# One attention, mixing and MLP kernel: the order of a batch's end, who adds the transform to x, where a row norm's inverse root stands, which engine step splits which weight when, and a 64-column transpose of the last key tile

## The reference

```
scores = q @ k.T / 8                      # 8 heads of 64, per batch
thresh = max(scores) - tau                # per row
attn   = softmax of the scores >= thresh  # sum + 1e-9 in the denominator
x      = attn @ v                         # heads side by side: 576 x 512

xk, xr = mu * x + (1 - mu) * x_prev       # x_prev: one position earlier
k = relu(xk @ w_k);  v = (k * k) @ w_v    # 512 -> 1024 -> 512
x = sigmoid(xr @ w_r) * v

u  = x + real(fft over positions of fft over channels of x)
un = (u - mean) / sqrt(var + 1e-6)        # per position, over channels
out = u + relu(un @ w_ch1) @ w_ch2        # 512 -> 2048 -> 512
```

## Time and profile before

| | |
|---|---|
| time, 3 runs | 1113.59, 1114.38, 1114.43 us (median 1114.38) |
| the profiled execution | 1115.46 us, its span 1113.7 us |
| PE busy | 1078.5 us (97%) |
| PEld busy | 1012.4 us (91%) |
| DVE, ACT, POOL busy | 551.7, 512.7, 420.0 us |
| mean granted TensorE clock | 0.988 |

### The profile page before, as it was taken

The page is one execution under the profiler, slowest core; times in us unless marked ns, Lnnn a source line. Parts: engine busy times, 40 slices in busy tenths (PEclk is TensorE's granted clock), DMA queues, the critical chain, the costliest instruction groups (busy, mean ns, idle before and its releaser), DMA issues.

```text
span 1113.7 us, 18462 instructions
## 1 busy us (share of the span) xinstructions
PE 1078.5 (97%) x7088; PEld 1012.4 (91%) x7088; DVE 551.7 (50%) x1081; ACT 512.7 (46%) x1250; POOL 420.0 (38%) x360
## 2 busy tenths in 40 slices
PE   7999999999999999999998999999999999999998
PEld 6899999998899998899997998888888888888998
DVE  7988764466565566565563655334114123223211
ACT  5979876646675646775644643221111111111110
POOL 5887653533663433763413445351111111111000
PEclk9989999999899999999999899999999999999999
DMA  8635111042121032121022207300200200200000
GB/s 237 176 98 170 37 43 34 24 140 53 65 56 35 23 104 89 66 57 34 2 71 77 105 1 287 122 1 1 69 1 1 69 1 1 68 1 1 35 1 33
DMA packets 37251, 69.30 MB, mean 62 GB/s; under 512 B 4134, under 2 KB 18604, under 8 KB 36140
## 3 DMA queue, kind: packets, MB, share of 16 engines
q1 hardware_dynamic: 36860, 67.80, 19.5%
q10 hardware_dynamic: 304, 0.33, 0.1%
HBM read 55.84 MB, written 12.28 MB: 61 GB/s over the span
## 4 chain that ended last, share of the span: by engine, by line
PE 82%; POOL 6%; DVE 4%; issue 3%; ACT 3%; DMA 0%; SPq 0%; DVEq 0%; POOLq 0%; ACTq 0%
PE PB L731 20%; PE PB L733 19%; PE PB L732 19%; PE PB L788 10%; PE PB L758 6%; PE PB L771 6%; POOL mix_l L630 1%; DVE probs L1284 1%; POOL x2T L662 1%; DVE neg_s L1270 1%; POOL q_hl L579 1%; POOL x2T L663 1%; POOL k_lo L571 1%; ACT exps L1019 1%; POOL fold_l L651 1%
## 5 line engine op out<-in xcount | busy, mean ns | idle before, releaser
L1228 ACT ACTIVATE h_hi<-PB 128x464 fp32r<-128x464 f32 (+1 forms) x80 | 44.5, 556 | 335.6 <-PE PB L733 335.6
L1461 DVE SCALAR_TENSOR_TENSOR h_lo<-PB,h_hi 128x464 fp32r<-128x464 f32 (+1 forms) x80 | 51.0, 638 | 264.0 <-ACT h_hi L1228 264.0
L788 PE MATMUL PB<-v_sb,probsT 128*128 128x64 f32 (+1 forms) x1440 | 180.2, 273 | 0.0
L788 PEld LDWEIGHTS PB<-v_sb,probsT 128*128 128x128 f32 x1440 | 175.1, 195 | 0.0
L1028 ACT ACTIVATE probsT<-PB 128x384 f32<-128x384 f32 (+1 forms) x288 | 109.5, 433 | 84.5 <-PE PB L771 83.5
L1284 DVE SCALAR_TENSOR_TENSOR probs<-neg_s,thresh,exps 128x576 f32<-128x576 f32 x144 | 145.7, 1012 | 0.3 <-PE PB L771 0.3
L1270 DVE TENSOR_SCALAR_CACHE_REDUCE neg_s<-PB,taus 128x576 f32<-128x576 f32 x144 | 117.1, 814 | 42.4 <-PE PB L758 38.1
L731 PE MATMUL PB<-un_h,w1h 128*128 128x464 f32 (+1 forms) x320 | 121.7, 380 | 0.0
L733 PE MATMUL PB<-un_h,w1l 128*128 128x464 f32 (+1 forms) x320 | 118.9, 371 | 0.0
L732 PE MATMUL PB<-h_lo,w2h 128*128 128x464 f32 (+1 forms) x320 | 118.8, 371 | 0.0
L731 PE MATMUL PB<-h_hi,w2h 128*128 128x464 f32 (+1 forms) x320 | 118.8, 371 | 0.0
(11 more groups left out here) (154 smaller groups left out, 2398.6 us busy)
## 6 DMA issues: line engine op xcount, KB each, us to landing
q_raw<-qT_dram SPq DMA_DIRECT2D x62, 160.0 KB, 3.2
k_raw<-kT_dram SPq DMA_DIRECT2D x64, 144.0 KB, 3.2
w_raw<-w_dram SPq DMA_DIRECT2D x8, 1024.0 KB, 9.3
cs<-cs_scr SPq DMA_DIRECT2D x4, 1740.0 KB, 8.0
u_scr<-x2T SPq DMA_DIRECT2D x4, 1152.0 KB, 5.2
cd<-cd_scr SPq DMA_DIRECT2D x4, 1032.0 KB
v_sb<-v_dram SPq DMA_DIRECT2D x16, 256.0 KB, 2.9
u_in<-u_scr SPq DMA_DIRECT2D x4, 928.0 KB, 6.1
```

The lines of the kernel that those rows point to most:

```text
L788: last = nc.tensor.matmul(bank(6 + p)[:, i * DH:i * DH + width], probsT[:, n % 2, kt * P128:(kt + 1) * P128], v_sb[:, kt, pair % 2, p * DH ...
L1461: nc.vector.scalar_tensor_tensor(h_lo[:, ft % 3, 0:w], bank(4 + ft % 3)[:, 0:w], 0.0, h_hi[:, ft % 3, 0:w].bitcast(F32), ALU.max, ALU.subt ...
```

## The change

1. **Short turn.** The last key tile is turned with 64 columns of probabilities as the stationary operand, not 128, into 64 partitions of PSUM. The other 64 partitions of that place are zeroed once, at the start; `probs` loses its columns of zeros. The moving operand stays the 128 columns of the identity.
2. **Row sums.** `rowsum` gets a second column that holds 1e-9, and the sum is a `tensor_reduce` where it was a `tensor_scalar`.
3. **Heads and splits.** `copy_head` stands one slot earlier. POOL's step for the low part of q comes before that of k, and the steps are spread over the slots in another way.
4. **First batch.** w_k's low part is made in eight halves over slots 17 to 35, no longer four pieces in slots 17, 21 and 22; the tables' pieces are one a slot; w_v is rounded in slots 36 to 43 (before: 28 to 35) and subtracted in slots 39 to 49.
5. **Shared sums.** DVE adds tiles 1 and 2 of the transform, POOL tiles 0 and 3. Two semaphores take the place of one.
6. **Order.** Y: `first_pair` of the first two groups stands ahead of their `second_pair`. `MIX_AT` has its gap one piece earlier (7 to 10 become 8 to 11); k starts in slot 13, no longer 12. In the drain x's last groups stand ahead of the fourth U group, and the reads and sums of U are later.
7. **Alone.** The inverse root stands after the second v group of the first half, the scaling after the fourth, `un_l` after the first v group of the second half; the low part of the first piece of w_2 stands right behind its high part.
8. **Start.** DVE prepares tau after it has split the first k and q, not before.

The core of the diff:

```diff
-MIX_AT = [3, 4, 5, 6, 7, 8, 9, 10, 12, 13, 14, 15, 17, 18, 19, 20]
+MIX_AT = [3, 4, 5, 6, 8, 9, 10, 11, 12, 13, 14, 15, 17, 18, 19, 20]
...
-            return 12 + (done + i * PARTS[stage] + part) * 23 // 36
+            return 13 + (done + i * PARTS[stage] + part) * 22 // 36
...
+        def add_dft(engine, tile, near, far):
+            engine.tensor_tensor(x2T[:, tile, 0:NYQ], x2T[:, tile, 0:NYQ], near[:, 0:NYQ], ALU.add)
+            return engine.tensor_tensor(x2T[:, tile, NYQ:S], x2T[:, tile, NYQ:S], far[:, NYQ - 2:0:-1], ALU.add)
...
+                            keys = min(P128, S - kt * P128)
+                            if n == 0 and keys < P128:
+                                pe.wait_ge(tail_zero, 1)
+                            last = nc.tensor.transpose(bank(4 + unit % 2)[0:keys, (kt - k0) * P128:(kt - k0 + 1) * P128],
+                                                       probs[:, n % 2, kt * P128:kt * P128 + keys], ident[:, :])
...
-                        if not alone(d):
+                        if not alone(d) and g == 1:
+                            second_pair(d, 0)
+                        if not alone(d) and g >= 1:
                             second_pair(d, g)
...
-                    if 0 <= n - 5 < TILES and (n - 5) % TILES_PAIR in (TAIL, TILES_PAIR - 1):
-                        copy_head(n - 5)
+                    if 0 <= n - 4 < TILES and (n - 4) % TILES_PAIR in (TAIL, TILES_PAIR - 1):
+                        copy_head(n - 4)
...
-                        nc.vector.tensor_scalar(rowinv[:, tiles], rowsum[:, tiles], EPS_SM, None, ALU.add).then_inc(sum_ready, 1)
+                        nc.vector.tensor_reduce(rowinv[:, tiles], rowsum[:, tiles, :], axis=AX.X, op=ALU.add).then_inc(sum_ready, 1)
...
+                    yield u_sum_at(d) + (0 if drains(d) else 1)
+                    dve.wait_ge(ab_ready, d * 2 + 2)
+                    add_dft(nc.vector, 1, diff[1], summ[1])
+                    yield u_sum_at(d) + (0 if drains(d) else 2)
+                    add_dft(nc.vector, 2, summ[1], diff[1]).then_inc(u_inner, 1)
```

More of the change, by code:

```diff
@@ L118, in u_at, with u_read_at, u_sum_at @@
     return U_AT_DRAIN if drains(d) else U_AT
+def u_read_at(d, pr):
+    return (40, 43)[pr] if drains(d) else U_AT[2 * pr + 1]
+def u_sum_at(d):
+    return 44 if drains(d) else U_AT[2]
 def stages(d):
@@ L156, in bank_turns @@
             of[group] = next(six)
+        elif drains(d) and stage == "u" and group[3] == 4:
+            of[group] = 4
         elif alone(d) or (drains(d) and stage == "u"):
@@ L211, in build @@
         thresh = m.put("thresh", [P128, 2 * TILES_PAIR], F32)
-        rowsum = m.put("rowsum", [P128, TILES_PAIR], F32)
+        rowsum = m.put("rowsum", [P128, TILES_PAIR, 2], F32)
         rowinv = m.put("rowinv", [P128, TILES_PAIR], F32)
@@ L239, in build @@
         v_sb = m.put("v_sb", [P128, KT, 2, 2 * DH], F32)
-        probs = m.put("probs", [P128, 2, KT * P128], F32)
+        probs = m.put("probs", [P128, 2, S], F32)
         probsT = m.put("probsT", [P128, 2, KT * P128], F32)
@@ L606, in setup_at @@
                         wr_low(2 * n - 23)
-                    if n == 17:
-                        wk_low(0)
-                        wk_low(1)
-                    if n in (21, 22):
-                        wk_low(n - 19)
-                    if n == 26:
-                        cd_low(0)
-                        cd_low(1)
-                    if n == 30:
-                        cs_low(0)
-                        cs_low(1)
-                    if n == 31:
-                        cs_low(2)
-                    if n in (35, 39, 40, 44):
-                        t = {35: 0, 39: 2, 40: 4, 44: 6}[n]
-                        wv_low(t)
-                        wv_low(t + 1)
+                    if n in WK_LOW_AT:
+                        for t, half in WK_LOW_AT[n]:
+                            wk_low(t, half)
+                    if n in (26, 27):
+                        cd_low(n - 26)
+                    if 28 <= n < 28 + ST:
+                        cs_low(n - 28)
+                    if n in WV_LOW_AT:
+                        for t in WV_LOW_AT[n]:
+                            wv_low(t)
                 def mixing(d):
@@ L1379, in dense @@
                                     split_w2(0, True)
[L1380 to L1384 removed]
+                                    split_w2(0, False)
                         if stage == "v":
@@ L1415, in dense @@
                     for pr in range(2):
[L1416 removed]
+                        yield u_read_at(d, pr)
                         dve.wait_ge(qcp_ready, d * 2 + pr + 1)
```

103 lines of the change are left out of this document (47 added, 56 removed).

## The result

The changed kernel takes 1105.56 us (median of five runs, 1105.26 to 1109.04) against 1114.43 (1113.59 to 1116.68). The ratio is 0.9923, 95% interval 0.9908 to 0.9938: 8.9 us faster, where I forecast 19.4. The time lies in the wider range on record (1086 to 1110), but outside the forecast's own (1087 to 1104), and next to the rival "the clock does not follow the waits" (1107). A run more than 1.5% above the fastest of its kernel counts as slow and is left out of medians and ratios; there is one, of part 7 alone.

What follows compares the result with a forecast made beforehand. The prediction took PE as the bound, with idle time and half clock to win. Terms -3.4 - 1.6 - 8.8 - 4 - 3.3 + 1.8 = -19.3 from 1115.46 gave 1096.2 profiled, 1095 median; own range 1087 to 1104.

Steps and rivals of the forecast that it cites:

- the clock does not follow the waits: Rival: half-clock stretches counted as won come back, elsewhere or in place; only -7.4 us, so 1107; chance 0.14.
- Row sums and first batch: First batch: shorter row sums halve probsT waits and remove a half-clock stretch, w_v roundings cost +2; net -3.4 us.
- Heads one slot earlier: Three PE waits for x_att go because the head copy stands a slot ahead: -1.6 us.
- Shared sums: Batches 1 and 2: 2.7 us waits for mix_l and the stretch at 289.8 go: -8.8 us.
- k one slot later: Slot 12 loses its dense product, so PE waits a little in three batches: +1.8 us.
- Drain: Drain: two mix_l waits and a half-clock stretch go, k's pieces come late: net -4 us, bounds 0 and -7.5.
- Short turn: Last key tile's turn with halved stationary columns: 0 us; rivals gave +26 for array switches or -6.8 for faster turns.
- Inverse root and split: Fourth batch: k_sql waits and the stretch at 675.5 go: -3.3 us, bounds 0 and -3.3.
- three signs of being wrong: PE's waits fall under 10 us, half-clock time stays near 27 us, or slots without waits change in length.

Runs made afterwards that it cites:

- part 7 alone: The kernel before with only part 7 of the change (root, scaling and splits of the fourth batch): 1110.98 us, ratio 1.0002.
- table-first kernel: The changed kernel with w_1's third and fourth pieces loaded behind the transform's table cs in the fourth batch, not ahead of it: 1098.97 us, ratio 0.9895.
- the variance later: The table-first kernel with PE's variance product and the root behind it one v group later in the fourth batch: 1096.68 us, ratio 0.9850.
- the kernel with the sums on POOL: The changed kernel with all four tiles of the transform added by POOL again: 1108.47 us, ratio 0.9945.

## Why the prediction was wrong

- *Row sums and first batch.* Right in size (waits for `probsT` -2.5, new ones for `probs` and `k_lo` +0.9, forecast -2; the stretch at 57.7 gone), wrong in cause: the held operation was real, and the new one takes 0.165 us as I took it, but that was worth about 0.9 us of PE's waits, and the rest of the change 1.7. The Trainium skill's rule that `tensor_reduce` never contends ("SBUF — State Buffer", section "Who interferes with whom") agrees with its 162 to 166 ns in all 32 sums. The roundings of w_v were put at +2; slots 36 to 47 did get 2.7 longer, and the run with w_v as before ties some 1.1 of it to w_v.
- *Heads one slot earlier.* Wrong: 0 for -1.6. The three waits for `x_att` became three for `xT`, 1.6 us as well.
- *Shared sums.* Right in size: the two stages get 9.1 us shorter, where my terms for them add up to 8.6. DVE's two tiles are worth 1.6 us a batch of it.
- *k one slot later.* Too high: PE's lead over the kernel before falls by no more than 0.2 us in the later slots of each batch, for 0.6.
- *Drain.* Right: -3.4 for -4; k's first group waits 3.4 us (2.5), and a stretch of 3.4 us lies on it.
- *Short turn.* Right: 0. The five turns take 0.545 us at the median of all 144 tiles, before and after. If 64 stationary columns count as another tiling mode, the drain that the Trainium skill's rule would bring ("TensorEngine Tiling (Array Packing)", section "Key Properties") doesn't show.
- *Inverse root and split.* **The step that failed.** Its own term was right (-3.0 for -3.3, with 1.0 more of wait for the variance in it). But I wrote of the stretch at 675.5 that it goes with its waits, and asked only whether DVE's moved work delays a v group. I didn't ask what a v that ends 3.9 us sooner meets: a table whose load starts at v's end, behind four loads that start at k's end. That made U's wait 1.2 us longer, and behind it came 17.1 us at half clock that cost 7.4: 8.6 us in all, a term that my sum had at nothing. The table-first kernel takes both away and gets 6.6 to 7.8 us; with the variance later the time is 1096.7, near the 1095 that I forecast for the change itself. Why this wait brings the half clock in every run of the changed kernel (twelve of twelve by their clocks), while waits as long in other kernels don't, stays open.
- *The rival.* "The half-clock stretches counted as won come back, elsewhere or in place" is what happened in size, and I gave it 0.14. The wait's place could have been read from the trace: U's start already waited 0.5 us, with `y_l` named as the releaser, though U's first product needs only the first `y_l`, done 1.8 us earlier.
- *The signs.* Of my three signs of being wrong one came (PE's waits fall by 7.2 us; I had set 10) and one nearly (23.9 us at half clock, 27.2 before). That the sum up to Y was right to half a microsecond is partly luck: the heads' missing 1.6 us and the 1.8 us that slot 12 did not cost cancel.

## What to carry to other kernels

When a stage gets shorter, list what is issued at its end and what is queued ahead of it on the transfer queue: the gain can come back as a wait for a transfer that was hidden by the slow stage. A short wait of PE can cost several times its length by the clock behind it (here 1.7 us, and 7.4 behind it); a few useless matmuls in such a wait show whether that is so, and may be a remedy. Compare kernels stage by stage at full clock before trusting a change of a few microseconds in the total, and measure what a stretch at half clock cost: one over a stage that waits for other engines cost nothing here.

## What the runs showed of the hardware that I had not expected

- 1.7 to 1.8 us of idle PE ahead of U were followed by 17.1 us at 1.2 GHz in both profiles of the changed kernel, 1.6 us by 13.7 in the kernel with the sums on POOL; in a wait of 3.6 us a stretch of 20.5 us began. 1.6 to 1.9 us in four other kernels were followed by none in the profiled execution. With 14 matmuls in the wait the clock stayed at 1.00.
- The same wait 1.7 us later brings two groups of times from one program, 1099 to 1101 and 1108 to 1112 us.
- 3.4 us at half clock in slots 36 to 47 cost nothing: the stage takes 41.5 us with it and without it.
- In the kernel before, a `tensor_scalar` over 128 x 4 or 128 x 5 elements takes 0.17 us in the 15 cases with no POOL instruction beside it, and 0.52 to 1.40 in the 17 with one. `tensor_reduce` over twice the elements takes 0.162 to 0.166 in all 32 of the changed kernel, 18 of them with one beside it.
- A turn with 64 stationary columns among turns with 128 costs no more than they do.
